# Attention, soft mixture and squared-ReLU layer on one core: the order of the first weight quarters

## The reference

```
q, k, v: (4, 8, 576, 64)                     # batch, heads, positions, head size
scores = q @ k.T / 8 + slope_h * -|i - j|     # kept where 0 <= i - j < 128
x = softmax(scores) @ v                      # -> 2304 tokens x 512
logits = x @ phi                             # 512 x 32 slots (8 experts x 4)
slot_in = softmax(logits over tokens).T @ x  # 32 x 512
slot_out = per expert: relu(slot_in @ w1) @ w2      # w1 512x1024, w2 1024x512
x = softmax(logits over slots) @ slot_out    # 2304 x 512
h = relu(x @ w_in)                           # w_in 512 x 2048
out = (h * h) @ w_out                        # w_out 2048 x 512, f32
```

## Time and profile before

| | us |
|---|---|
| median of 3 runs | 403.23 (402.55 to 403.57) |
| profiled execution | 402.54 |
| its span, first to last instruction | 400.7 |
| TensorE busy | 388.4 (97%) |
| VectorE busy | 283.5 (71%) |
| ScalarE busy | 264.4 (66%) |
| GpSimd busy | 97.9 (24%) |

### The profile page before, as it was taken

The page is one execution under the profiler, slowest core; times in us unless marked ns, Lnnn a source line. Parts: engine busy times, 40 slices in busy tenths (PEclk is TensorE's granted clock), DMA queues, the critical chain, the costliest instruction groups (busy, mean ns, idle before and its releaser), DMA issues.

```text
span 400.7 us, 8879 instructions
## 1 busy us (share of the span) xinstructions
PE 388.4 (97%) x3316; PEld 320.1 (80%) x3316; DVE 283.5 (71%) x741; ACT 264.4 (66%) x609; POOL 97.9 (24%) x94
## 2 busy tenths in 40 slices
PE   7699999999999999999899999999999999999997
PEld 6478888787877654444578888889999999999996
DVE  5788888888872655023899994658786978777752
ACT  4989899898972421001875877858877767777720
POOL 4687777868661010000053000000000000000000
PEclk9999999999999999999999999999999999999999
DMA  6688899989698479999900101001010101001011
GB/s 193 174 304 252 250 319 245 311 252 262 191 290 284 150 272 334 404 386 386 374 7 1 54 0 52 2 0 54 0 55 2 54 0 52 0 0 52 2 52 54
DMA packets 50021, 61.39 MB, mean 153 GB/s; under 512 B 25536, under 2 KB 33728, under 8 KB 48320
## 3 DMA queue, kind: packets, MB, share of 16 engines
q1 hardware_dynamic: 49440, 60.37, 45.3%
q10 hardware_dynamic: 544, 0.52, 0.4%
HBM read 56.16 MB, written 4.72 MB: 152 GB/s over the span
## 4 chain that ended last, share of the span: by engine, by line
PE 84%; DVE 5%; ACT 4%; DMA 4%; issue 1%; POOL 1%; SPq 1%; POOLq 0%; DVEq 0%
PE psum L1597 9%; PE psum L1598 9%; PE psum L1599 9%; PE psum L1315 6%; PE psum L1271 6%; PE psum L1297 6%; PE psum L1571 4%; PE psum L1572 4%; PE psum L1573 4%; DMA win_sb<-in_moe_w_in 4%; PE psum L1472 3%; PE psum L1583 3%; PE psum L1493 2%; PE psum L1230 2%; PE psum L1383 2%; ACT probs L1004 2%
## 5 line engine op out<-in xcount | busy, mean ns | idle before, releaser
L897 DVE TENSOR_TENSOR step_lo<-step_raw,step_hi 128x896 fp32r<-128x896 f32 x48 | 50.2, 1088 | 25.5 <-ACT step_hi L1140 25.4
L1004 ACT ACTIVATE probs<-probs,row_min 128x256 f32<-128x256 f32 (+1 forms) x128 | 60.0, 471 | 12.0 <-DVE row_min L642 12.0
L584 POOL TENSOR_TENSOR probs<-probs,row_inv 128x1024 f32<-128x1024 f32 x31 | 59.1, 1928 | 23.5 <-DVE row_inv L693 23.5
L1597 PE MATMUL psum<-t_hi,step_hi 128*128 128x256 f32 x192 | 53.8, 280 | 0.1
L1599 PE MATMUL psum<-t_hi,step_lo 128*128 128x256 f32 x192 | 53.7, 280 | 0.0
L1598 PE MATMUL psum<-t_lo,step_hi 128*128 128x256 f32 x192 | 53.7, 279 | 0.0
L1140 ACT CAST step_hi<-step_raw 128x896 fp32r<-128x896 f32 x48 | 42.8, 944 | 7.1 <-DVE step_raw L910 6.7
L1152 ACT ACTIVATE step_raw<-psum 128x512 f32<-128x512 f32 x48 | 26.0, 595 | 28.8 <-PE psum L1583 24.9
L642 DVE CUSTOM_DVE_ANT_0 probs<-psum,rel 128x256 f32<-128x256 f32 (+1 forms) x128 | 42.0, 385 | 2.9 <-PE psum L1271 2.8
L1599 PE MATMUL psum<-wout_hi,step_lo 128*128 128x256 f32 x144 | 40.3, 280 | 0.0
L1597 PE MATMUL psum<-wout_hi,step_hi 128*128 128x256 f32 x144 | 40.2, 280 | 0.0
(11 more groups left out here) (183 smaller groups left out, 858.1 us busy)
## 6 DMA issues: line engine op xcount, KB each, us to landing
ring<-in_moe_w SPq DMA_DIRECT2D x16, 1024.0 KB, 6.3
ring<-in_moe_w SPq DMA_DIRECT2D x4, 2048.0 KB, 11.8
q_raw<-in_q SPq DMA_DIRECT2D x16, 256.0 KB, 3.5
v_in<-in_v SPq DMA_DIRECT2D x32, 128.0 KB, 2.8
ring_x<-in_moe_w SPq DMA_DIRECT2D x2, 2048.0 KB, 8.3
win_sb<-in_moe_w_in SPq DMA_DIRECT2D x4, 1024.0 KB, 12.3
wout_raw<-in_moe_w_out SPq DMA_DIRECT2D x4, 1024.0 KB, 14.5
out_x<-out_sb SPq DMA_DIRECT2D x8, 512.0 KB, 2.8
```

The source lines that it names most:

```text
L584: nc.gpsimd.tensor_tensor(probs[:, par, h, 0:4, :], probs[:, par, h, 0:4, :], row_inv[:, par, 4 * h:4 * h + 4].unsqueeze(2).to_broadcast([ ...
L897: nc.vector.tensor_tensor(step_lo[j][:, i, 1:8, :], step_raw[j][:, i, 1:8, :], step_hi[j][:, i, :, :].bitcast(F32), ALU.subtract).then_inc ...
L1004: nc.scalar.activation(t, t, ACT.Exp, bias=row_min[:, par, one:one + 1], scale=-1.0, accum_out=row_sum[:, par, one:one + 1]).then_inc(exp_ ...
L1597: mm(to, hi, w_hi, start=clears, stop=False, skip_group_check=True)
```

## The change

SP issues the loads as w_in 0, w_in 1, w_out 0, w_in 2, w_out 1, w_in 3, w_out 2, w_out 3. TensorE does projections 0 and 1 between mix sums and mix parts of the third and fourth quarter; on ScalarE and VectorE the first splits move ahead of take_mix(0), and those of the later quarters go between hidden steps. The fourth quarter of the mix is taken behind low_part(5) on VectorE and high_part(5) on ScalarE. soT gets a place of its own, since it is now read while relu_h is written, and the parts of quarter 2 use PSUM bank 6 with their sum in bank 7, since bank 2 and 3 are then in use by hidden steps.

```diff
--- before.py
+++ after.py
@@ -189,7 +189,6 @@
         lg = sb("lg", [P, QT * B, NS])
         comb_st = sb("comb_st", [P, 4, QT * B])
         siT = sb("siT", [P, DC, NS])
-        soT = sb("soT", [P, DC, NS])
         assert place["at"] <= late_at
 
         place["at"] = att_at + 4 * 2 * F1
@@ -206,6 +205,8 @@
         assert place["at"] <= late_at
         place["at"] -= 4 * 2 * 2 * FT
         relu_h = sb("relu_h", [P, 2, 2 * FT])
+        soT = sb("soT", [P, DC, NS])
+        assert place["at"] <= late_at
 
 
         BLOCK = 4 * KH * NH
@@ -526,10 +527,14 @@
 
             sp.wait_ge(e1_done, IN_X[1] // 2 + 1)
             sp.wait_ge(e2_done, IN_X[0] // 2 + 1)
-            for i in range(4):
-                load_win(i)
-            for i in range(4):
-                load_wout(i)
+            load_win(0)
+            load_win(1)
+            load_wout(0)
+            load_win(2)
+            load_wout(1)
+            load_win(3)
+            load_wout(2)
+            load_wout(3)
 
             def store(n, par):
                 if isinstance(n, int) and n < CONV:
@@ -946,32 +951,37 @@
 
             def first():
                 take_part(1)
+                split_low(0)
                 take_mix(0)
                 take_mix(1)
-                take_part(3)
                 low_part(0)
-                split_low(0)
-                take_mix(2)
                 low_part(1)
                 split_low(1)
+                low_part(2)
+
+            def first_group():
+
+                take_mix(2)
+                split_low(2)
+                low_part(3)
+                take_part(3)
+                low_part(4)
+                split_low(4)
+                low_part(5)
                 take_mix(3)
+                low_part(6)
+                split_low(6)
+                low_part(7)
 
             def step(n, par):
                 if isinstance(n, int) and n < CONV:
                     for u in range(FU):
                         m = FU * n + AHEAD + u
-                        if m < FU:
-                            if u == 0:
-                                for u2 in range(2, AHEAD):
-                                    low_part(u2)
-                                    if u2 not in LOWS_OF_POOL:
-                                        split_low(u2)
+                        if m == AHEAD:
+                            first_group()
+                        elif FU <= m < FU * CONV:
                             low_part(m)
-                            if m not in LOWS_OF_POOL:
-                                split_low(m)
-                        elif m < FU * CONV:
-                            low_part(m)
-                        elif AHEAD_STEPS[u] is not None:
+                        elif m >= FU * CONV and AHEAD_STEPS[u] is not None:
                             next_steps(CONV, AHEAD_STEPS[u])
                         for work, half, t in T_OF_DVE.get((n, u), ()):
                             (form_t, low_t)[work](half, t)
@@ -1169,30 +1179,40 @@
 
             def first():
                 take_part(0)
+                split_high(0)
                 take_mix(0)
-                take_part(2)
                 take_mix(1)
                 high_part(0)
-                split_high(0)
+                high_part(1)
+                take_part(2)
+                split_high(1)
+                high_part(2)
+
+            def first_group():
+
+                split_high(2)
                 take_mix(2)
-                high_part(1)
-                split_high(1)
+                split_high(3)
+                high_part(3)
+                split_high(4)
+                high_part(4)
+                split_high(5)
+                high_part(5)
                 take_mix(3)
+                split_high(6)
+                high_part(6)
+                split_high(7)
+                high_part(7)
 
             def step(n, par):
                 if isinstance(n, int) and n < CONV:
                     for u in range(FU):
                         m = FU * n + AHEAD + u
-                        if m < FU:
-                            if u == 0:
-                                for u2 in range(2, AHEAD):
-                                    high_part(u2)
-                                    split_high(u2)
+                        if m == AHEAD:
+                            first_group()
+                        elif FU <= m < FU * CONV:
                             high_part(m)
-                            split_high(m)
-                        elif m < FU * CONV:
-                            high_part(m)
-                        elif AHEAD_STEPS[u] is not None:
+                        elif m >= FU * CONV and AHEAD_STEPS[u] is not None:
                             next_steps(CONV, AHEAD_STEPS[u])
                         for half, t in T_OF_ACT.get((n, u), ()):
                             high_t(half, t)
@@ -1655,31 +1675,31 @@
                 mix_parts(0)
                 mix_parts(1)
                 mix_sum(0)
-                mix_parts(2)
                 mix_sum(1)
-                mix_parts(3)
                 pe.wait_ge(mix_ready, 1)
                 hidden(0, 0, 0)
-                mix_sum(2)
                 hidden(0, 1, 1)
-                mix_sum(3)
+                mix_parts(2)
                 pe.wait_ge(mix_ready, 2)
                 hidden(0, 2, 2)
 
             def first_step():
                 project(0, 0, 0, 0)
+                mix_sum(2)
+                hidden(0, 3, 3)
+                project(0, 1, 1, 0)
+                mix_parts(3)
                 pe.wait_ge(mix_ready, 3)
-                hidden(0, 3, 3)
                 hidden(0, 4, 4)
-                project(0, 1, 1, 0)
+                project(0, 2, 2, 0)
                 hidden(0, 5, 5)
-                project(0, 2, 2, 0)
+                mix_sum(3)
+                project(0, 3, 3, 0)
                 pe.wait_ge(mix_ready, 4)
                 hidden(0, 6, 6)
-                project(0, 3, 3, 0)
                 hidden(0, 7, 7)
+                project(0, 4, 4, 0)
                 hidden(1, 8, 0)
-                project(0, 4, 4, 0)
                 hidden(1, 9, 1)
                 project(0, 5, 5, 0)
                 hidden(1, 10, 2)
@@ -1710,7 +1730,7 @@
 LG_PIECES = (((0, 0, 2 * P), (2, 0, S // 2 - 2 * P)), ((2, S // 2 - 2 * P, P), (3, 0, P), (4, 0, TAIL)))
 L2_BANKS = ((4, 5), (6, 7))
 TURN_BANKS = (1, 0)
-MIX_BANKS = ((6, 7), (0, 4), (2, 3), (6, 7))
+MIX_BANKS = ((6, 7), (0, 4), (6, 7), (6, 7))
 LOWS_OF_POOL = (3, 5, 7)
 SQ_OF_DVE = FU + AHEAD
 SQ_ACT_AT = FU * CONV - SQ_OF_DVE - NB * CONV + 1
```

## The result

The changed kernel is slower: 407.61 us (median of 20 runs, 405.96 to 410.91) against 403.4 (20 runs), ratio 1.0086 with a 95% interval of 1.0065 to 1.0107, which is 3.5 us. The ratio isn't that of the two medians, which lie 4.2 apart. The forecast was 405.7, which is 2.5 over the median of 403.23 known then, with a range of 403.4 to 407.0. Ratio times 403.23 gives 406.7, inside the range; the plain median of the change lies 0.6 above its upper end. The profiled execution took 407.25. In three of the later sets one execution stands far above all the others (484.91, 551.67 and 770.31 us): the medians count it, the ratios leave it out.

What follows compares the result with a forecast made beforehand. TensorE, busy 388.4 of 400.7 us, was taken as the bound. Front nets 0.1; a 2.6 us pause before hidden 6 puts the eighth projection at 221.0 against 218.61: +2.4, taken as +2.5 on 403.23, giving 405.7; range 403.4 to 407.0.

Steps and rivals of the forecast that it cites:

- The front gives back what it wins: TensorE's front: project 0 starts 2.0 us earlier, but work moved behind it leaves 0.1 us at the eighth projection.
- The port: VectorE beside GpSimd's weight split: square(3) and square(4) held, each near 2.8 us; 0.69 alone.
- The queue ahead of take_mix(3): VectorE reaches take_mix(3) behind newly placed operations, ending 211.35; TensorE pauses 2.6 us ahead of hidden 6.
- Rival D: TensorE behind the new pause: clock falls to half, one or two projections take 2.75 us more, 408.5 to 411; chance 0.07.
- The base: Whole kernel: count from the median of runs, 403.23 us, since the profiled execution, 402.54, lies 0.7 below it.

Runs made afterwards that it cites:

- own_splits: Changed kernel with its order kept, but VectorE does the low splits of u = 3, 5 and 7 and GpSimd none: 403.69 us, ratio 0.9993 to before.
- before_own: Kernel before the change, with all low splits of w_out on VectorE and none on GpSimd: 403.02 us, ratio 0.9999.
- old_loads: Changed kernel's programs, but loads in the order of before (w_in 0 to 3, then w_out 0 to 3): 415.11 us, ratio 1.0283 to before.
- late_pool5: Changed kernel, but GpSimd's split for u=5 also waits until the fourth mix quarter is ready: 404.8 us, ratio 1.0011 to before.
- reordered kernel: Changed kernel reordered: take_mix(0) before the first split, hidden 2 behind projection 0, VectorE does split 3, GpSimd's split 5 waits for the mix: 403.38 us, ratio 0.9998.
- reorder_holds: Reordered kernel, with GpSimd's splits as in the changed one (u = 3, 5, 7, each once the high half stands): 404.36 us, ratio 1.0046 to before.
- mix3_first: Changed kernel with take_mix(3) ahead of low_part(5) on VectorE: 406.01 us, ratio 1.0047 to before.
- after: Profiled execution of the changed kernel itself, nothing further edited: 407.25 us.
- fill_pause: Changed kernel with 18 idle transposes on TensorE in the back pause, the one ahead of hidden 6: 407.01 us, ratio 1.0086 to before.

## Why the prediction was right, step by step

From the first mix product (185.53 in the profile forecast from, 186.41 in the one after):

| | forecast | measured |
|---|---|---|
| ScalarE's split_high(0) starts | 2.9 | 2.5 |
| hidden 0 | 6.0 | 5.6 |
| projection 0 | 8.7 | 8.2 |
| square(3), square(4) on VectorE, long | 2.8 both | 2.88, 2.89 |
| take_mix(3) ends | 25.8 | 25.7 |
| pause ahead of hidden 6 | 2.6 | 2.6 between matmuls, 3.0 as the wait of the weight load |
| hidden 6 | 25.9 | 25.8 |
| hidden 6 to the eighth projection | 9.6 | 11.15 |
| eighth projection | 35.5 | 36.9 |

The mechanism came as forecast: a hold of two squares and a longer queue ahead of take_mix(3). That the end of take_mix(3) agrees within 0.1 is partly luck. Hidden 0 came 0.4 sooner than forecast, and the stretch from it to the end of take_mix(3) took 20.1 where the forecast had 19.9.

- **The front gives back what it wins**: shown by own_splits and before_own, two orders without holds whose eighth projections stand within 0.1 us in one profile each; of the 2.0 us nothing shows in the time of own_splits, whose interval leaves room for a gain of 1.5. w_out 0 landed 0.4 earlier against the first mix product than forecast in this profile (2.5 to 3.9 in the other profiles with the new order of loads), and old_loads shows that it counts one for one.
- **The port**: shown. late_pool5 moves one GpSimd operation and takes 2.8 us off the median. The prediction left open whether anything but the square is held. In the reordered kernels low parts (2.77, 2.78) and a split (3.42) are, and a copy out of PSUM is not (0.69 at 207.83). So the rule of the Trainium skill (SBUF — State Buffer, section "SBUF: two separate sides") holds for all three forms. The engine that comes second waits for what is left of the other's operation, so the price depends on the moment: a square took 2.89 when both began together, 2.27 and 1.87 when it came later (reorder_holds, late_pool5).
- **The queue ahead of take_mix(3)**: shown by mix3_first, 1.3 us of TensorE's wait for 1.45 us of passed work. The list of what is newly ahead of it was wrong in two places: take_part(3) stood ahead of it before too, and low_part(2) and split_low(2) are new. The sum is untouched, since it counts VectorE's program in its actual order.
- **Rival D was under-weighted and its size was off.** It had 0.07. The mean clock was below 1 in 12 of 20 runs, and in the profiled one it fell behind the pause. There the two hidden steps took 1.02 for 0.46 and projection 4 took 3.7 for 2.75, together 1.5 us, not the 2.75 to 5.5 assumed: it was back at full rate within some 3 us, after five matmuls of the projection. The argument that a pause of 1.6 us had not cost clock said nothing about one of 3 us. This is most of what makes +3.5 out of the forecast +2.5: the changed kernel's runs at full clock (median 406.29) lie 2.8 over those of before (403.45 to 403.56 in the four later sets, whose clocks are on record).
- **The base**: the profile of before was an early one (402.54, the lowest of its runs), and counting from the median instead was right.

## What to carry to other kernels

Before GpSimd is given work to unburden VectorE, look at what VectorE does beside it: here a split that GpSimd took over held VectorE for up to 2.2 us (1.2 and 1.6 where VectorE's operation came later), where the split itself would have cost it 1.14. When a step is moved forward in one engine's program, look for what now stands behind it: the 2.0 us won at the first projection were work moved behind it, and the price was paid by the fourth quarter's take_mix, which had six more calls of VectorE's program ahead of it (low_part 2 to 5, split_low 2 and 4). And price a pause of TensorE of about 3 us above its length, since the matmuls behind it may run at half rate for a while, in some runs and not in others. Its length alone doesn't decide: waits of 3.0 and 2.9 us were followed by a fall (after, fill_pause), while waits of 3.4 and 3.6 us at the front were not (mix3_first, late_pool5; clock 1.00 from 192 to 198 us in both).

## What the runs showed of the hardware that was not expected

The same program loses clock in some runs and not in others: 12 of 20 runs of the changed kernel had a mean clock below 1, 6 of 12 with the back pause filled, 1 of 6 with both filled. The kernel before, whose longest pause in the passage is 1.6 us, had it in 6 of 29, 1 of 21, 7 of 23 and 2 of 23 runs of its four sets. So not every fall belongs to the passage. The profile of reorder_holds (mean clock 0.992) shows one that doesn't. Its windows in the attention, and its first mix product:

```profile
18.00:20.00 2.00, 0.93 (x5) 0.59 0.28 75
20.00:22.00 2.00, 2.00 (x11) 0.50 0.53 137
...
24.00:26.00 2.00, 2.00 (x16) 0.71 0.92 364
...
189.53 1.05 PE L1557 MATMUL psum<-win_sb,soT 128*32 128x512 f32 x6
```

The clock falls near 18 us, where TensorE is busy for 0.93 of 2 us, and is back by 26. In the profile of before the neighbouring stretch is as empty (busy for 0.40 of the 2 us from 16 to 18), and the clock stays at 1.00. The passage starts at 189.53 here, 2.5 us or more later than in every other profile (185.53 to 187.00), and the clock is 1.00 throughout it. The kernel before has runs of 0.990 to 0.992 that take some 3 us more too; that they fell at the same place is likely and not shown, since none of them was profiled.

And the hold of VectorE by GpSimd does not depend on which VectorE operation with two SBUF inputs it meets: where GpSimd's operation gets its turn just ahead of VectorE's, the square takes 2.89, the low part 2.78, a split 3.42, each its own time and 2.1 to 2.2 us.
